# Top-32 attention with two feed-forward layers on one core: the exponential taken of all scores, the selection and its sum made by VectorE afterwards, the first chunk's last tile closed early

## The reference, cut to what matters

```
# attention: batch 4, 8 heads, 576 positions, head size 64, float32
scores = scale * q @ k.T
kth    = 32nd largest score of each row
scores = where(scores >= kth, scores, -1e9)
attn   = exp(scores - max(scores))
attn   = attn / (sum(attn) + 1e-9)
x      = attn @ v                        # -> 2304 tokens x 512
# layer 1
h = x @ w_in;  g = max(0.01*h, h);       x = g @ w_out      # 512 -> 2048 -> 512
# layer 2
h = x @ w_in;  g = 0 if h<=-1, h if h>=1, else (h+1)**2/4;  out = g @ w_out
```

## Time and profile before

| | |
|---|---|
| median of 3 runs | 1221.04 us (1219.96 to 1221.80) |
| the profiled execution | 1223.14 us |
| its span, first to last instruction | 1221.2 us |
| mean granted TensorE clock | 0.961 |
| busy: PE, DVE, ACT, POOL | 1120.3, 930.0, 701.9, 608.5 us |
| PE weight load busy | 1008.9 us |

### The profile page before, as it was taken

How to read it: one execution, slowest core, us unless ns; L and a number is a source line. 1 busy time by engine, 2 the same in 40 slices (tenths; PEclk the granted TensorE clock), 3 DMA queues, 4 the chain that set the end, 5 groups by cost and what they waited for, 6 DMA issues and landing times.

```text
span 1221.2 us, 21057 instructions
## 1 busy us (share of the span) xinstructions
PE 1120.3 (92%) x7360; PEld 1008.9 (83%) x7360; DVE 930.0 (76%) x2088; ACT 701.9 (57%) x1577; POOL 608.5 (50%) x582
## 2 busy tenths in 40 slices
PE   3456998979999999999999989999899999999998
PEld 2334887869889888888987968888789999999998
DVE  7999999979889999899988988969989105300244
ACT  5566777646667765666666665665765524322232
POOL 5666878735446644555545653444745423222221
PEclk9667999979999999999998989999999999999999
DMA  6787997856675687767676656445445667787764
GB/s 223 280 304 255 370 340 292 273 188 210 214 245 208 237 284 276 254 244 247 223 238 206 223 181 220 164 167 189 156 173 196 210 241 258 249 278 255 245 240 147
DMA packets 86504, 287.12 MB, mean 235 GB/s; under 512 B 9600, under 2 KB 13184, under 8 KB 86400
## 3 DMA queue, kind: packets, MB, share of 16 engines
q1 hardware_dynamic: 78912, 270.04, 64.3%
q10 hardware_dynamic: 7488, 15.73, 3.7%
HBM read 247.46 MB, written 38.27 MB: 234 GB/s over the span
## 4 chain that ended last, share of the span: by engine, by line
PE 69%; DVE 18%; POOL 4%; ACT 4%; issue 3%; DMA 0%; ACTq 0%; POOLq 0%
PE ps_f L746 19%; PE ps_f L748 17%; PE ps_f L747 17%; DVE top L971 7%; DVE work L974 6%; PE ps_av L709 6%; DVE part_r L998 3%; PE ps_s L665 3%; PE ps_t L686 2%; PE ps_t L692 2%; PE ps_t L665 1%; DVE drop L980 1%; POOL gate L588 1%; POOL part_o L594 1%; POOL drop L573 1%
## 5 line engine op out<-in xcount | busy, mean ns | idle before, releaser
L746 PE MATMUL ps_f<-gate,w_ring 128*128 128x384 f32 (+2 forms) x896 | 290.5, 324 | 22.5 <-POOL gate L588 20.6
L971 DVE MAX8 top<-work 128x8 f32<-128x576 f32 x432 | 309.1, 742 | 0.1
L746 PE MATMUL ps_f<-xy,w_ring 128*128 128x384 f32 (+2 forms) x896 | 289.7, 323 | 9.1 <-POOL xy L598 6.1
L573 POOL TENSOR_TENSOR drop<-scores,drop 128x576 f32<-128x576 f32 x144 | 207.9, 1444 | 165.7 <-DVE drop L980 165.7
L748 PE MATMUL ps_f<-gate,w_ring 128*128 128x384 f32 (+2 forms) x896 | 282.1, 315 | 0.0
L747 PE MATMUL ps_f<-gate,w_ring 128*128 128x384 f32 (+2 forms) x896 | 282.0, 315 | 0.0
L748 PE MATMUL ps_f<-xy,w_ring 128*128 128x384 f32 (+2 forms) x896 | 280.6, 313 | 0.0
L747 PE MATMUL ps_f<-xy,w_ring 128*128 128x384 f32 (+2 forms) x896 | 280.5, 313 | 0.0
L974 DVE MATCH_REPLACE8 work<-top,work 128x576 f32<-128x576 f32 x288 | 212.7, 738 | 0.0
L746 PEld LDWEIGHTS ps_f<-gate,w_ring 128*128 128x128 f32 x896 | 171.1, 191 | 40.1 <-POOL gate L588 22.2
L746 PEld LDWEIGHTS ps_f<-xy,w_ring 128*128 128x128 f32 x896 | 169.8, 190 | 27.8 <-issue 10.4
(11 more groups left out here) (88 smaller groups left out, 1835.6 us busy)
## 6 DMA issues: line engine op xcount, KB each, us to landing
w_ring<-w_split SPq DMA_DIRECT2D x412, 512.0 KB, 4.1
w_split<-w_ring SPq DMA_DIRECT2D x36, 512.0 KB, 6.3
raw<-wd SPq DMA_DIRECT2D x64, 256.0 KB, 4.9
w_split<-xy SPq DMA_DIRECT2D x28, 512.0 KB, 3.8
kq<-kqd ACTq DMA_DIRECT2D x12, 576.0 KB, 6.2
v_sb<-vd ACTq DMA_DIRECT2D x12, 320.0 KB, 4.0
kq<-kqd SPq DMA_DIRECT2D x4, 576.0 KB, 6.4
out_t<-y_acc ACTq DMA_DIRECT2D x12, 192.0 KB, 3.4
```

The source lines that it names most:

```text
L573: pool.tensor_tensor(slot, scores[:, it.n % S_SLOTS, t - it.first, :], slot, ALU.add).then_inc(masked, 1)
L746: pe.matmul(out, w[:, 0, m], high, start=b == 0, stop=False)
L971: dve.max(top[:, t % T_SLOTS, 8 * r:8 * r + 8], source(t, r)).then_inc(dve_step, 1)
```

## The change

The exponential is taken of all scores, into a new buffer `expo`, as soon as the row's maximum is known; it has no row sum. `find_drop` and GpSimd's `mask` are gone. In their place VectorE's `keep` compares the scores with the 32nd largest value, multiplies by the exponential and writes the tile together with its row sum. `keep` waits for the exponential of its tile, and for the transposes of the item before the last. `EXP_LAG` goes from 5 to 3, `INV_LAG` from 3 to 2, and an item's output step from its last tile's number + 7 (6 in the first chunk) to + 5 (4). So READY is 20 for the first chunk and 150 for the last; the units in each step are the same, two steps earlier. The sum is closed and inverted ahead of VectorE's second part of the step, no longer at its end. `finish_first` finishes tile 15, the last of the first chunk, before VectorE goes on with tile 16. The 28 pieces are prepared two to a step, the eight direct stores come two to a step from step 17. The first pair's keys and its first 256 query columns are loaded ahead of the rest, and the first item's copy of scores goes tile by tile. `copy_values` writes the high part first, x_raw behind it. A product's order becomes weight high by high, weight low by high, weight high by low, with a wait for the high part ahead of it and one for the low part ahead of the third matmul.

```diff
-EXP_LAG = 5
-MASK_LAG = 4
-INV_LAG = 3
+EXP_LAG = 3
+KEEP_LAG = 4
+INV_LAG = 2
...
 def out_step(it):
-    return it.last + (6 if starts_early(it.gp) else 7)
+    return it.last + (4 if starts_early(it.gp) else 5)
...
-    s = 5 * (s - PREP_FROM)
-    return range(max(0, s // 3), max(0, min(len(PREP), (s + 5) // 3)))
+    s = 2 * (s - PREP_FROM)
+    return range(max(0, s), max(0, min(len(PREP), s + 2)))
...
-            def mask(t):
-                it = ITEM_OF[t]
-                pool.wait_ge(dropped, t + 1)
-                slot = drop[:, t % D_SLOTS, :]
-                pool.tensor_tensor(slot, scores[:, it.n % S_SLOTS, t - it.first, :], slot, ALU.add).then_inc(masked, 1)
...
-                    pe.matmul(out, w[:, 0, m], high, start=b == 0, stop=False)
-                    pe.matmul(out, w[:, 0, m], low, start=False, stop=False)
-                    mm = pe.matmul(out, w[:, 1, m], high, start=False, stop=end)
+                    opens = u.i == 0 and not (u.hidden and u.block)
...
+                    pe.matmul(out, w[:, 0, m], high, start=first, stop=False)
+                    pe.matmul(out, w[:, 1, m], high, start=False, stop=False)
+                    if opens and u.hidden and not u.layer:
+                        pe.wait_ge(x_low_done, gp + 1)
+                    elif opens and u.hidden:
+                        pe.wait_ge(y_low_done, Y_OF[u.chunk.n, b].y + 1)
+                    elif opens:
+                        pe.wait_ge(gate_low_done[u.layer], source.in_layer + 1)
+                    mm = pe.matmul(out, w[:, 0, m], low, start=False, stop=end)
...
                 act.wait_ge(neg_max_ready, t + 1)
-                act.wait_ge(masked, t + 1)
-                need(act, transposed, it.n - P_SLOTS + 1)
-                act.activation(probs[:, it.n % P_SLOTS, a * S:(a + 1) * S], drop[:, t % D_SLOTS, :], ACT.Exp,
-                               bias=neg_max[:, t % 8:t % 8 + 1], scale=SCALE,
-                               accum_out=row_sum[:, it.n % T_SLOTS, a:a + 1]).then_inc(exp_done, 1)
+                need(act, kept, t - D_SLOTS + 1)
+                act.activation(expo[:, t % D_SLOTS, :], scores[:, it.n % S_SLOTS, t - it.first, :], ACT.Exp,
+                               bias=neg_max[:, t % 8:t % 8 + 1], scale=SCALE).then_inc(exp_done, 1)
...
-            def find_drop(t):
-                need(dve, exp_done, t - D_SLOTS + 1)
+            def keep(t):
                 it = ITEM_OF[t]
-                dve.tensor_scalar(drop[:, t % D_SLOTS, :], scores[:, it.n % S_SLOTS, t - it.first, :],
-                                  top[:, t % T_SLOTS, TOP_K - 1:TOP_K], DROPPED, ALU.is_lt,
-                                  ALU.mult).then_inc(dropped, 1)
+                a = t - it.first
+                dve.wait_ge(exp_done, t + 1)
+                need(dve, transposed, it.n - P_SLOTS + 1)
+                dve.scalar_tensor_tensor(out=probs[:, it.n % P_SLOTS, a * S:(a + 1) * S],
+                                         in0=scores[:, it.n % S_SLOTS, a, :],
+                                         scalar=top[:, t % T_SLOTS, TOP_K - 1:TOP_K], in1=expo[:, t % D_SLOTS, :],
+                                         op0=ALU.is_ge, op1=ALU.mult,
+                                         accum_out=row_sum[:, it.n % T_SLOTS, a:a + 1]).then_inc(kept, 1)
...
+            def finish_first(t, count):
+                top8(t - 1, 2)
...
+                drop8(t - 1, 2)
...
+                top8(t - 1, 3)
...
+                keep(t - 1)
...
+                top8(t, 0)
...
+                close_sum(ITEM_OF[t - 1])
+                drop8(t, 0)
...
+                invert_sum(ITEM_OF[t - 1])
...
```

More of the change, by code:

```diff
@@ L201, in score_step @@
 def score_step(it):
-    if it.first < READY[0]:
-        return max(0, it.first - 2, ITEMS[it.n - S_SLOTS].last + EXP_LAG if it.n >= S_SLOTS else 0)
+    if it.first <= READY[0]:
+        return max(0, it.first - 2, ITEMS[it.n - S_SLOTS].last + KEEP_LAG if it.n >= S_SLOTS else 0)
     return it.first - it.mixed
@@ L341, in item_closing @@
     for it in ITEMS:
-        if it.last + INV_LAG - starts_early(it.gp) == t:
+        if it.last != FIRST_END and it.last + INV_LAG == t:
             return it
@@ L382, in build @@
         neg_max = sb("neg_max", [P, 8])
-        drop = sb("drop", [P, D_SLOTS, S])
+        expo = sb("expo", [P, D_SLOTS, S])
         probs = sb("probs", [P, P_SLOTS, 2 * S])
@@ L632, in _ @@
                     low_x(CHUNKS[0].last_gp)
-                if s < READY[0] and s >= MASK_LAG:
-                    mask(s - MASK_LAG)
                 if s - 2 in VALUES_AT and s < READY[0]:
@@ L654, in score @@
             def score(it):
-                if it.rows in (0, 2):
+                if it.n == 0:
+                    pe.wait_ge(kq_first, 32)
+                elif it.rows == 2 or it.rows == 0 and it.gp:
                     pe.wait_ge(kq_loaded[it.pair], 16 * (it.b + 1))
@@ L733, in products @@
                     w = w_ring[:, g % W_SLOTS, :, :]
+                    first, end = b == 0, b == u.sources - 1
                     if u.hidden:
-                        if not u.layer and not u.block and u.i == 0:
-                            pe.wait_ge(x_low_done, u.chunk.last_gp - CK + 1 + b + 1)
-                        if u.layer and not u.block and u.i == 0:
-                            pe.wait_ge(y_low_done, Y_OF[u.chunk.n, b].y + 1)
                         high, low, out = x_of(u.chunk, 0, b), x_of(u.chunk, 1, b), as_x(u.chunk, bank(u))
@@ L772, in _ @@
                     feed(u)
+                if s - 1 in VALUES_AT and s < READY[0]:
+                    values(VALUES_AT[s - 1])
                 if s == READY[0] - 1:
@@ L778, in _ @@
                     transpose(OUT_AT[s])
-                if s in VALUES_AT and s < READY[0]:
+                if s == READY[0] - 1:
                     values(VALUES_AT[s])
@@ L804, in copy_scores @@
                 if it.n >= S_SLOTS:
-                    act.wait_ge(masked, ITEMS[it.n - S_SLOTS].last + 1)
+                    act.wait_ge(kept, ITEMS[it.n - S_SLOTS].last + 1)
                 dst = scores[:, it.n % S_SLOTS, :, :]
+                if it.n == 0:
+                    for a in range(2):
+                        for j, src in enumerate(score_halves(it)):
+                            act.wait_ge(scores_done, j + 1)
+                            op = act.activation(dst[:, a, j * PART:(j + 1) * PART], src[:, a, 0:PART], ACT.Copy)
+                        op.then_inc(scores_copied, 1)
+                    return
                 for j, src in enumerate(score_halves(it)):
@@ L1052, in _ @@
                     last_top = count
-                soon = shut and shut.last == LAST_OF_GROUP[CHUNKS[0].last_gp]
-                if soon:
-                    close_sum(shut)
-                    count += 1
                 if new:
@@ L1060, in _ @@
                     count += 1
-                if soon:
-                    dve.wait_ge(dve_step, count - 1)
-                    invert_sum(shut)
                 for u in third:
                     event(u)
-                if shut and not soon:
-                    close_sum(shut)
-                    count += 1
                 if old:
                     dve.wait_ge(dve_step, last_top)
-                    find_drop(t - 1)
-                if shut and not soon:
-                    dve.wait_ge(dve_step, count)
-                    invert_sum(shut)
+                    keep(t - 1)
 _INS = ["kqd", "vd", "wd"]
```

73 lines of the change are left out of this document (54 added, 19 removed).

## The result

The changed kernel takes **1260.54 us** (median of 4, 1259.46 to 1260.96) against 1221.42 us for the one before in the same call (1219.96 to 1222.59): a ratio of 1.0319, 95% interval 1.0304 to 1.0335. It is **39 us slower**; 8 us faster was forecast, and the range ended at 1236.

The account below looks back on a forecast made before the run. VectorE was taken to set the pace up to 110 us, then TensorE, VectorE close behind. Start -5, TensorE's waits -10 and VectorE's load +7 made -8: median 1213 us, range 1200 to 1236.

Parts of the forecast that it names:

- The price of `keep`: VectorE, each tile: 0.73 us in place of 0.43, +0.30 us free of interference, 43 us over 144 tiles.
- Rival three: VectorE's `keep` runs at half rate: 0.60 us more a tile, some +80, 1300 us; chance 0.03.
- The interference: VectorE meeting GpSimd: `keep`'s 19 us nearly cancels against savings from masks gone; near 0, between -10 and +20.
- The start: Up to the first product with the last low part: tile 16 at 100.5, product at 114.2, 5 us gained.
- The waits for low parts: TensorE's 22 waits for GpSimd's low parts: 10 us gained, 6 by matmul order and 4 by masks gone.
- What VectorE's load gives back: After 110 us, 46 turns paced by VectorE alone cost between 0 and 17 us; 7 us taken.
- the deeper couplings go the same way: `normalise` waits for a same-step inversion with bank reads behind, `keep` for exponential and transposes; inside the 7 us.
- rival one: VectorE becomes the pace: 17 us from turns, 6 from closes waiting on ScalarE; +15, 1236 us; chance 0.24.
- it decides from where VectorE passes 97%: The VectorE share, from 110 us to the end of attention, above which VectorE becoming the pace decides.
- TensorE's idle time over 50 us: Sign of being wrong: TensorE idles more than 50 us from the first low-part product to attention's end; under 35 expected.
- the start later than 118 us: Sign of being wrong: the first product with the last low part after 118 us; near 114 expected.
- Rivals two and four: Two: low-part waits vanish nearly whole, -25, 1196, chance 0.15; four: ScalarE's weight loads prevent an earlier start, -3, 0.11.

Follow-up runs that it names:

- before_order: The kernel before with only the new order of a product's three matmuls and the new waits for high and low part: 1213.87 us (0.9937).
- probs4: The changed kernel with four `probs` buffers in place of three, two for expo and one for x_raw: 1260.63 us (1.0329).
- norm_late: The changed kernel with ScalarE's `normalise` moved from ahead of a step's second units to behind the third: 1219.13 us (0.9989).
- norm_late_light: norm_late with `keep` as a one-input operation without a sum, selection left out, sum taken with the exponential: 1203.23 us (0.9855).
- heavy_drop: The kernel before with `find_drop` as a two-input operation with a sum, the masking's effect left out: 1242.26 us (1.0174).
- light `keep`: The changed kernel with `keep` as a one-input operation, selection left out, sum taken by ScalarE's exponential: 1235.38 us (1.0123).
- before_order_start: before_order with the changed kernel's first loads, tile-by-tile copy of the first item's scores, and high part ahead of x_raw: 1212.72 us (0.9939).
- close_now: The changed kernel with the sum closed and inverted right behind the `keep` of an item's last tile: 1234.38 us (1.0095).
- before_order_norm_late: before_order with ScalarE's `normalise` moved from ahead of a step's second units to behind the third: 1229.35 us (1.0074).

## Why the prediction was wrong, point by point

**The price of `keep` was right.** VectorE's timeline of the changed kernel with GpSimd idle:

```profile
404.22 0.83 DVE L1000 SCALAR_TENSOR_TENSOR probs<-scores,top,expo 128x576 f32<-128x576 f32 x1
404.95 0.10 DVE L1000 DVE_READ_ACCUMULATOR probs<-scores,top,expo 128x1 f32 x1
404.95 0.78 DVE L989 MAX8 top<-scores 128x8 f32<-128x576 f32 x1
```

0.73 us from start to start, for 0.43 before; whole unhindered turns take 5.61 us for 5.30, with a close 5.73 to 5.75. Of the two parts I added, 0.66 and 0.07, the pass alone is 0.73 and the read starts together with the next instruction; the sum was right, the split was not. Rival three is refuted: no half rate with two float32 inputs and a sum. The statement in the Trainium skill, "Vector Engine (DVE) Microarchitecture Reference", section "Points that are easy to get wrong", that this form runs at half throughput, is contradicted by these 0.73 us for 576 columns.

**The interference was right.** All of `keep` and of the layer-2 operation, from the changed kernel's groups (busy us, mean ns, idle before):

```profile
L1000 DVE SCALAR_TENSOR_TENSOR probs<-scores,top,expo 128x576 f32<-128x576 f32 x144 | 129.9, 902 | 2.0 <-DVE work L992 1.2
L1020 DVE SCALAR_TENSOR_TENSOR part_r<-part_r 128x384 f32<-128x384 f32 (+2 forms) x112 | 64.9, 579 | 90.4 <-ACT part_o L902 90.4
```

144 at an undisturbed 0.80 would be 115, so 15 us are interference (19 forecast for 127 of them); the layer-2 operations take 64.9 us for 74.8 before the change, 9.9 saved (10 forecast).

**The start was near.** Tile 16 starts at 104.56, not 100.5, 4 us beyond the forecast. The first product:

```profile
115.23 0.39 PE L752 MATMUL ps_f<-xy,w_ring 128*128 128x256 f32 x1 [0.47 <-ACT xy L879]
115.45 0.28 PE L753 MATMUL ps_f<-xy,w_ring 128*128 128x256 f32 x1
116.31 0.39 PE L760 MATMUL ps_f<-xy,w_ring 128*128 128x256 f32 x1 [0.58 <-POOL xy L582]
```

Its low part is used at 116.31 for 119.40: 3 us gained, 5 forecast. But before_order, whose attention steps are those of before, has that matmul at 116.82, and its tile 16 starts 1.1 us earlier than before's though nothing that it does up to there was edited (its first MAX8 comes at 7.70 for 8.00). So the rest of the start's changes, tile 15's early finish and `keep`'s load together, is worth 0.5 us net, which single executions cannot show; probs4, with the same steps as the changed kernel, has that matmul at 113.70 and ends no earlier.

**The waits for low parts were right.** 8 us by before_order (6 forecast for it). In the changed kernel the wait for the gate's low part fell to 13.3 us in 13, as forecast near 12, and from 100 us on all listed waits for GpSimd fell by 12.0 us (10 forecast). But the waits for ScalarE rose by 30.8, so this gain did not show in the sum.

**The step that failed is "What VectorE's load gives back", +7.** It held two things, and both were mis-sized. First the load: from 46 turns in which VectorE alone paces I took 7 us, with an upper end of 17. The runs give 16 (norm_late against norm_late_light), 21 (heavy_drop) and 25 (in the changed kernel) for the whole; my term was for the steps behind the start only, and between tiles 16 and 143 it is 10.7, 17.1 and 22.8. Without the tie (the first two) that is up to my upper end, above what I took; with the tie it is beyond the upper end. That I counted only turns that were already short, and a longer turn makes further ones VectorE's, would explain this, but was not tested. Second, "the deeper couplings go the same way": I saw that `normalise` would wait for an inversion in the same step with bank reads behind it, and forecast the wait at over 40 us. I put it inside the 7, and at 6 us in rival one. It is **41 us** in the changed kernel (32 with the light `keep`), and put alone into the kernel before it costs 38.3 us between tiles 16 and 143. Load and tie together are 57 us, the loss is 39: the rest gave 18 back, of which 8 are the order, its part of the start included. About 10 stay for masks gone, two steps fewer and the start's other changes. norm_late_light against before_order_start, 9.5 us, agrees; no run takes these apart. From tile 143 to the end it is 8 to 13 us less than before in the runs with the changed kernel's output steps.

**Rival one had the side and a wrong sign to look for.** It named both mechanisms, but as VectorE becoming full: "it decides from where VectorE passes 97%". VectorE went down to 89.5%. Two engines that wait for each other in most turns show as idle time on both. So my reading that 5% of idle time is room said nothing: in the changed kernel part of it was waiting on the partner, which norm_late's 93.4% with the same instructions shows. Of the signs of being wrong, TensorE's idle time over 50 us did come, with 60.9 us from 110 to 955 us; the start later than 118 us did not. ScalarE's wait, forecast at over 40 us, was 199.9. The 57 closes counted in rival one were too few: from 110 us on there are 72 inversions. Rivals two and four did not occur.

**Left open.** How each us of ScalarE's wait turns into TensorE's idle time is shown here by single cases and by the sums; and the changed kernel with the old order of matmuls was not run. About 10 of the 39 us are longer TensorE busy time in the two profiled executions: the clock granted from 300 to 955 us is 0.97 for 0.99, and norm_late has 0.99 again. Over whole runs the mean clocks of the two kernels overlap (0.958 to 0.965, and 0.959 to 0.972 before), so this share is rough.

## What to carry to other kernels

When producer and consumer of a small value sit in in-order queues of two engines, keep a distance between them, and when a change closes it, price it by everything that is queued behind the waiting instruction and comes back to the producer: here one call's place was worth 38 to 41 us with all instructions unchanged. How much distance is enough was not the same everywhere: half a step left 29 us of wait before, and 109 in close_now. When busy shares fall on two engines at once although one got more work, look for such a ring before calling the idle time room. And take a large change apart: its one free part, the order of three matmuls, was worth 8 us, and was hidden in a loss of 39; but a wait made shorter did not always pay: in before_order_norm_late it shrank by 25 us and the kernel lost 15.5.

## What the runs showed of the hardware

Reading out VectorE's sum adds no time behind the pass: the read at 404.95 and the next MAX8 at 404.95 start together. The pass is 0.73 us where MAX8's over the same columns is 0.67 (404.95 to 405.62); whether the sum makes that difference no run shows. Closing the sum straight behind it does cost time: in close_now 315.41, 315.53, 315.73, 315.81 for three dependent small instructions. And a two-input operation meets GpSimd even when that is busy for only a third of the time: `keep` over the whole changed kernel, minimum, median and maximum in ns, and one that began beside a GpSimd operation:

```profile
L1000 DVE SCALAR_TENSOR_TENSOR probs<-scores,top,expo x144: 802/818/1879, 15.4 to 995.1; 128x576 f32<-128x576 f32 x144
...
189.96 1.48 POOL L576 TENSOR_TENSOR w_ring<-raw,w_ring 128x512 fp32r<-128x512 f32 x1
190.21 1.84 DVE L1000 SCALAR_TENSOR_TENSOR probs<-scores,top,expo 128x576 f32<-128x576 f32 x1
```
